# First product in plain float32 with attention between its parts, gates by tanh, mixes in pairs

## What is computed

```python
# attention: keys of the last 128 positions
scores = where(mask, scale * q @ k.T + bias, -1e9)
attn = exp(scores - max(scores)); attn = attn / (sum(attn) + 1e-9)
x = attn @ v                                # (4, 576, 512) after joining the heads
# first block, w_in 512 x 1024, w_out 1024 x 512
h = maximum(x @ w_in, 0)
gate = 1 / (1 + exp(-conv3(h)))             # 3 taps around each position
x2 = (h * gate) @ moe_w_out
# second block, w_val and w_out 512 x 512
gate2 = 1 / (1 + exp(-causal_conv5(x2)))    # 5 taps, own and four before
y = (gate2 * (x2 @ w_val)) @ moe2_w_out
```

## Time and profile before

| | |
|---|---|
| median of 3 runs | 470.3 us |
| profiled execution, its own time | 470.26 us |
| its span, first to last instruction | 468.5 us |
| mean granted TensorE clock | 0.978 |
| PE, DVE, ACT, POOL busy | 94%, 68%, 63%, 18% |
| chain that ended last | PE 81%, DVE 7%, ACT 5% |

### The profile page before, as it was taken

How to read it: one execution, slowest core, us unless ns; L and a number is a source line. 1 busy time by engine, 2 the same in 40 slices (tenths; PEclk the granted TensorE clock), 3 DMA queues, 4 the chain that set the end, 5 groups by cost and what they waited for, 6 DMA issues and landing times.

```text
span 468.5 us, 9674 instructions
## 1 busy us (share of the span) xinstructions
PE 442.6 (94%) x3376; PEld 410.3 (88%) x3376; DVE 320.3 (68%) x1128; ACT 297.1 (63%) x916; POOL 82.3 (18%) x116
## 2 busy tenths in 40 slices
PE   4888579997999999999999999999999999999997
PEld 3668558996889998999889998999889998899997
DVE  7795895976685767757776667847778475847760
ACT  3686953386667975398566976488666876377132
POOL 3310990044000220013000230014000140004000
PEclk9999857999999999999999999999999999999999
DMA  8865102001211012011210112121211100010002
GB/s 212 222 199 214 45 15 78 1 1 45 69 47 38 25 46 68 27 49 46 70 45 27 37 25 67 37 62 42 57 45 44 36 2 1 2 50 2 1 14 88
DMA packets 38928, 25.81 MB, mean 55 GB/s; under 512 B 22752, under 2 KB 35040, under 8 KB 38880
## 3 DMA queue, kind: packets, MB, share of 16 engines
q1 hardware_dynamic: 38880, 25.20, 18.7%
HBM read 20.47 MB, written 4.72 MB: 54 GB/s over the span
## 4 chain that ended last, share of the span: by engine, by line
PE 81%; DVE 7%; ACT 5%; issue 2%; DMA 1%; POOL 1%; SPq 1%; DVEq 0%; ACTq 0%
PE bank L827 20%; PE bank L828 20%; PE bank L829 20%; PE bank L808 8%; PE bank L778 8%; PE bank L788 6%; DVE probs L597 1%; DMA k_all<-k_t 1%; DVE probs L565 1%; ACT conv L468 1%; DVE gate L706 1%; DVE conv L650 1%; DVE w_lo L620 1%; ACT conv L474 1%; ACT bank L459 1%
## 5 line engine op out<-in xcount | busy, mean ns | idle before, releaser
L827 PE MATMUL bank<-g_hi,w_hi 128*128 128x288 f32 x384 | 121.2, 316 | 0.0
L827 PE MATMUL bank<-x_hi,w_hi 128*128 128x290 f32 (+1 forms) x384 | 114.3, 298 | 3.7 <-DVE x_lo L640 1.4
L828 PE MATMUL bank<-g_lo,w_hi 128*128 128x288 f32 x384 | 114.0, 297 | 0.0
L828 PE MATMUL bank<-x_lo,w_hi 128*128 128x290 f32 (+1 forms) x384 | 113.6, 296 | 0.0
L829 PE MATMUL bank<-g_hi,w_lo 128*128 128x288 f32 x384 | 113.6, 296 | 0.0
L829 PE MATMUL bank<-x_hi,w_lo 128*128 128x290 f32 (+1 forms) x384 | 113.3, 295 | 0.0
L389 POOL TENSOR_TENSOR g_lo<-conv,g_hi 128x288 fp32r<-128x288 f32 x64 | 51.9, 812 | 330.7 <-ACT g_hi L482 330.7
L650 DVE SCALAR_TENSOR_TENSOR conv<-bank,taps,conv 128x288 f32<-128x288 f32 (+1 forms) x128 | 65.5, 513 | 53.6 <-ACT conv L468 53.4
L420 ACT ACTIVATE probs<-probs,neg_max 128x192 f32<-128x192 f32 (+2 forms) x144 | 62.0, 432 | 28.9 <-DVE neg_max L565 28.4
L827 PEld LDWEIGHTS bank<-x_hi,w_hi 128*128 128x128 f32 x384 | 72.4, 188 | 4.6 <-DVE conv L658 1.8
L827 PEld LDWEIGHTS bank<-g_hi,w_hi 128*128 128x128 f32 x384 | 72.8, 190 | 0.8 <-issue 0.5
(11 more groups left out here) (49 smaller groups left out, 542.9 us busy)
## 6 DMA issues: line engine op xcount, KB each, us to landing
w_raw<-panels SPq DMA_DIRECT2D x12, 512.0 KB, 5.9
y_t<-y_sb SPq DMA_DIRECT2D x32, 144.0 KB, 1.7
q_tile<-q_t SPq DMA_DIRECT2D x32, 128.0 KB, 3.0
k_all<-k_t SPq DMA_DIRECT2D x16, 256.0 KB, 3.7
v_tile<-v_tiles SPq DMA_DIRECT2D x16, 256.0 KB, 2.7
q_tile<-q_t SPq DMA_DIRECT2D x8, 64.0 KB, 2.4
k_all<-k_t SPq DMA_DIRECT2D x4, 128.0 KB, 2.6
v_tile<-v_tiles SPq DMA_DIRECT2D x4, 128.0 KB, 3.0
```

The source lines that it names most:

```text
L827: pe.matmul(out, w_hi[:, p, col:col + P], hi(k), start=start, stop=False)
L828: pe.matmul(out, w_hi[:, p, col:col + P], lo(k), start=False, stop=False)
```

## The change

Four things are done.

*First product of chunk 0.* It multiplies the unrounded rows (`x_raw`, in the place of `x_lo`) by the unrounded weights (`w_raw`) in plain float32: 32 matmuls of 290 columns for 96 float32r ones. The first three tiles are copied to `x_raw` by ACT and not split. POOL no longer rounds panels 0 to 3 at the start, and DVE splits no weights in steps. The splits come later: ACT rounds the 98 columns of rows that both chunks read (`seam_high`, beat 10) and the four panels (`w_in_high`, 1024 columns each, beats 12 to 15), POOL keeps the rests (`seam_low`, `w_in_low`, 16 pieces). POOL rounds panels 4 to 7 in beats 0 to 3, DVE keeps their rests in halves in beats 1 to 8; panels 8 and 9 are split by POOL behind the up weights, 10 and 11 in beats 10 and 14 of chunk 1.

*Attention in the up beats.* Steps 12 to 18 of batch 0 go into beats 1 to 7 of chunk 0, step 19 into beat 12. The up product of chunk 0 uses banks 0 to 3 in turn (each waits for the gated rows four groups back); its down product makes the first parts of all four groups, then the second parts.

*Gates by tanh.* The sigmoid of z is (1 + tanh(z/2))/2: `Relu` takes a scale of 0.5 (which halves h, and so z), the gate is `Tanh`, the multiplication adds 1 in a two-operation instruction; the second gate has its scale in the activation, and the output copy takes a scale of 0.5.

*Mixes in pairs.* `probs_t` has four buffers, and PE's close does nothing at even steps and two mixes at odd ones.

```diff
+T_RING = 4
+WOVEN = 7
+PLAIN = 3
+SEAM = SEQ - READ
...
+        x_raw = nc.alloc_sbuf_tensor_at("x_raw", [P, KM, SEQ], F32, offset=base + x_raw_at)
-        probs_t = [place(f"probs_t{r}", [P, 4 * P]) for r in range(2)]
+        probs_t = [place(f"probs_t{r}", [P, 4 * P]) for r in range(T_RING)]
...
+        def up_bank(c, m):
+            return UP_BANK[m] if c > 0 else m % KM
+        def down_of(c, j):
+            n = j - DOWN0
+            if c == 0 and n < KM:
+                return n % 2, n // 2
+            return n // 2, n % 2
...
+            if c == 0 and KW - WOVEN <= j < KW:
+                return FIRST + j - KW + WOVEN
+            if c == 0 and j == DOWN0:
+                return STEPS - 1
...
-                    if c == 0 and j == VAL0 + 2:
-                        run(slot, close, range(FIRST, STEPS))
...
@@ on POOL @@
             def beat(c, j, step):
+                if c == 0 and j < P_VAL - P_OUT:
+                    round_panel(P_OUT + j)
                 if c < CHUNKS and 2 <= j < KW + 2:
                     g1_low(c, j - 2)
-                if c == 0 and j < KW and j % 2 == 1:
-                    round_panel(P_OUT + j // 2)
-                if c == 0 and j in (DOWN0, DOWN0 + 4):
-                    split_panel(P_VAL + (j - DOWN0) // 4)
-                if c == 1 and j in (0, 4):
-                    split_panel(P_OUT2 + j // 4)
-
-            for n in range(P_OUT):
-                round_panel(n)
+                if c == 0 and j == KW + 2:
+                    seam_low()
+                if c == 0 and DOWN0 <= j < DOWN0 + P_OUT:
+                    w_in_low(j - DOWN0)
+                if c == 0 and j in (DOWN0 + P_OUT, DOWN0 + P_OUT + 1):
+                    split_panel(P_VAL + j - DOWN0 - P_OUT)
+                if c == 1 and j in (KW + 2, KW + 6):
+                    split_panel(P_OUT2 + (j - KW) // 4)
...
@@ on ACT @@
+            def seam_high():
+                act.wait_ge(up_done, KW)
+                act.copy(x_hi[:, :, SEAM:PLAIN * P], x_raw[:, :, SEAM:PLAIN * P]).then_inc(seam_rounded, 1)
+            def w_in_high(n):
+                act.wait_ge(up_done, KW)
+                act.wait_ge(panel_loaded[n], 16)
+                act.copy(w_hi[:, n, :], w_raw[:, n, :]).then_inc(w_in_rounded, 1)
...
-                act.activation(bank[:, 0:READ], bank[:, 0:READ], ACT.Relu).then_inc(hidden_done, 1)
+                act.activation(bank[:, 0:READ], bank[:, 0:READ], ACT.Relu, scale=0.5).then_inc(hidden_done, 1)
...
-                               ACT.Sigmoid).then_inc(gate1_done, 1)
+                act.activation(conv[n % DEPTH][:, :], conv[n % DEPTH][:, :], ACT.Tanh).then_inc(gate1_done, 1)
...
@@ on DVE @@
-                dve.tensor_tensor(conv[n % DEPTH][:, :], banks[UP_BANK[m]][:, at:at + HALF],
-                                  conv[n % DEPTH][:, :], ALU.mult).then_inc(g1_done, 1)
+                dve.scalar_tensor_tensor(out=conv[n % DEPTH][:, :], in0=conv[n % DEPTH][:, :], scalar=1.0,
+                                         in1=banks[up_bank(c, m)][:, at:at + HALF], op0=ALU.add,
+                                         op1=ALU.mult).then_inc(g1_done, 1)
...
-                if 0 <= step - STEPS + 2 * P_VAL < 2 * P_VAL:
-                    low_of_panel(step - STEPS + 2 * P_VAL)
...
+                if c == 0 and 1 <= j < 1 + 2 * (P_VAL - P_OUT):
+                    low_of_panel(j - 1)
...
@@ on PE @@
+            def close(step):
+                if step % 2 == 1:
+                    mix(step - 1)
+                    mix(step)
...
+                    if c == 0:
+                        if m == 0:
+                            pe.wait_ge(panel_loaded[P_IN + k], 16)
+                        last = pe.matmul(banks[bank][:, 0:READ], w_raw[:, P_IN + k, m * P:m * P + P],
+                                         x_raw[:, k, at:at + READ], start=first, stop=final)
...
-            walk(slot, mix, beat)
+            walk(slot, close, beat)
```

More of the change, by code:

```diff
@@ L242, in last_of_run @@
         def last_of_run(step):
-            return step % STEPS in (FIRST - 1, STEPS - 1)
+            return step % STEPS in (FIRST - 1, STEPS - 1) and step != FIRST - 1
         def chunk_of(step):
@@ L425, in slot, with turned_rows @@
             def slot(step):
+                turned_rows(step)
+                if step + LOOK - 1 < ALL_STEPS:
+                    exps(step + LOOK - 1)
+            def turned_rows(step):
                 _, t, _ = where(step)
                 act.wait_ge(turned, step + 1)
-                reach(act, mixed, step - 1)
-                to = probs_t[step % 2]
+                reach(act, mixed, step - T_RING + 1)
+                to = probs_t[step % T_RING]
                 if 0 < t < FULL:
@@ L505, in out_rows @@
                 reach(act, y_stored[n % Y_RING], 16 * (n // Y_RING))
-                act.copy(y_sb[n % Y_RING][:, :], banks[out_bank(c, m)][:, 0:HALF]).then_inc(y_kept, 1)
+                act.activation(y_sb[n % Y_RING][:, :], banks[out_bank(c, m)][:, 0:HALF], ACT.Copy,
+                               scale=0.5).then_inc(y_kept, 1)
             def beat(c, j, step):
-                if step is not None:
+                if step is not None and j < KW:
+                    turned_rows(step)
+                elif step is not None:
                     slot(step)
@@ L516, in beat @@
                     gate_rows(c, j - 1)
+                if step is not None and j < KW:
+                    exps(step + LOOK - 1)
                 if c < CHUNKS and 2 <= j < KW + 2:
                     g1_high(c, j - 2)
+                if c == 0 and j == KW + 2:
+                    seam_high()
+                if c == 0 and DOWN0 <= j < DOWN0 + P_OUT:
+                    w_in_high(j - DOWN0)
                 if c > 0 and 0 <= j - VAL0 < KM:
                     g2_high(c - 1, j - VAL0)
-                if c < CHUNKS and DOWN0 <= j < OUT0 and j % 2 == 1:
-                    x2_high(c, (j - DOWN0) // 2)
+                if c < CHUNKS and DOWN0 <= j < OUT0 and down_of(c, j)[1] == 1:
+                    x2_high(c, down_of(c, j)[0])
                 if out_of(c, j):
@@ L631, in slot @@
                 scores(kept_early(step), 1)
-                if 0 <= step - STEPS + 2 * P_VAL < 2 * P_VAL:
-                    low_of_panel(step - STEPS + 2 * P_VAL)
             def close(step):
                 _, t, hp = where(step)
-                if hp == PAIRS - 1:
+                if hp == PAIRS - 1 and step // PAIRS >= PLAIN:
                     w = width_of(t)
@@ L674, in val_rows @@
                 dve.wait_ge(gate2_done, n + 1)
-                dve.tensor_tensor(gate2[:, m, :], banks[val_bank(c, m)][:, 0:HALF], gate2[:, m, :],
-                                  ALU.mult).then_inc(g2_done, 1)
+                dve.scalar_tensor_tensor(out=gate2[:, m, :], in0=gate2[:, m, :], scalar=1.0,
+                                         in1=banks[val_bank(c, m)][:, 0:HALF], op0=ALU.add,
+                                         op1=ALU.mult).then_inc(g2_done, 1)
             def g2_low(c, m):
@@ L796, in mix @@
                     pe.wait_ge(v_loaded[tile % V_RING], 16 * (tile // V_RING + 1))
-                    reach(pe, x_lo_done, tile)
+                    tiles_left(tile)
                 pe.wait_ge(copied, step + 1)
@@ L867, in up @@
                     pe.wait_ge(y_kept, KM * (c - 2) + OUT_BANK.index(bank) + 1)
-                product(banks[bank][:, 0:READ], lambda k: (P_IN + k, m * P),
-                        lambda k: x_hi[:, k, at:at + READ], lambda k: x_lo[:, k, at:at + READ],
-                        range(KM)).then_inc(up_done, 1)
+                for k in range(KM):
+                    first, final = k == 0, k == KM - 1
+                    if c == 0:
+                        if m == 0:
+                            pe.wait_ge(panel_loaded[P_IN + k], 16)
+                        last = pe.matmul(banks[bank][:, 0:READ], w_raw[:, P_IN + k, m * P:m * P + P],
+                                         x_raw[:, k, at:at + READ], start=first, stop=final)
+                    else:
+                        if c == 1 and m == 0:
+                            pe.wait_ge(w_in_split, (k + 1) * (PANEL // PIECE))
+                        last = product(banks[bank][:, 0:READ], lambda k: (P_IN + k, m * P),
+                                       lambda k: x_hi[:, k, at:at + READ], lambda k: x_lo[:, k, at:at + READ],
+                                       [k], first=first, final=final)
+                last.then_inc(up_done, 1)
             def val(c, m):
@@ L931, in beat @@
                 if c < CHUNKS and DOWN0 <= j < OUT0:
-                    down(c, (j - DOWN0) // 2, (j - DOWN0) % 2)
+                    down(c, *down_of(c, j))
                 if out_of(c, j):
```

62 lines of the change are left out of this document (40 added, 22 removed).

## The result

| | before | changed |
|---|---|---|
| median | 470.31 us (4 runs, 468.93 to 470.8) | 453.83 us (4 runs, 453.49 to 454.09) |
| profiled execution, own time | 470.26 us | 453.9 us |
| its span | 468.5 us | 452.0 us |
| mean granted TensorE clock | 0.978 | 1.0 |

The ratio is 0.9686 (95% interval 0.9648 to 0.9723): 3.1% faster. The forecast was 448.5 us, with a range of 443 to 457.

The account below looks back on a forecast made before the run. TensorE, busy 94% of the span, bounds it; gains come from its empty time before 121 us or its own sequence. 12.9 + 0 + 9.0 = 21.9 us off 470.26 gave 448.4, forecast 448.5 us, range 443 to 457.

Parts of the forecast that it names:

- part 5: Later batches: pairing removes 30 mix blocks at 0.30 us each, 9.0 us in full; bounds 0 and 9.6.
- Part 1: First run of 12 steps: eight steps save 3.5 us, 0.7 more before the product; up product starts at 33.5 us.
- Part 2: Up product with seven steps woven in: 27 us at 3.55 us per beat, from a two-beat loop of 7.1 us.
- The rival of contention: Woven beats: DVE stops beside POOL, 4.5 us per beat instead of 3.55; 457 us in all, chance 0.17.
- Part 3: First chunk's down product: 16.6 us with a 2.5 us wait for step 19's copies; second chunk starts at 77.1.
- Part 4: Second chunk: a new lag as large as the present 2.8 us idle time; change 0, bounds +2 and -2.8.
- The second rival: Later batches: pairing gives little, the extra returns at the turn or a PE wait opens; 454.5 us, chance 0.11.
- The hidden parts: Two-input gating, table loads, scales in activations and four small memsets: hidden; PE does not wait for the loads after 121 us.
- The slower rival: Woven beats: the loop closes in one beat, 7.1 us each, 24.9 us more; 473 us, chance 0.04.

Follow-up runs that it names:

- run 7: Changed kernel with two of four plain matmuls left out in groups 1 to 7 of the first chunk's up product: 452.09 us.
- run 6: Changed kernel with DVE's subtraction of the down weights put ahead of the taps in chunk 0's woven beats: 453.35 us.
- run 8: Changed kernel with POOL's low halves of the gated rows in chunk 0 cut to 16 of 288 columns: 454.46 us.
- run 3: Changed kernel with DVE's subtraction of rows (`x_lo`) issued one slot later, at the next step's close: 451.81 us.
- run 2: Changed kernel with the pairs undone, one mix at each step again: 457.44 us.
- run 4: Changed kernel with sigmoid gates and plain multiplication in place of the tanh gates: 471.51 us.
- run 12: Changed kernel with rows subtracted one slot later, weight subtraction ahead of the taps, and mixes of steps 18 and 19 one beat later: 447.82 us.
- run 10: Changed kernel with the three edits of run 12 plus POOL's low pieces of the first weights made by columns over all four panels: 451.82 us.
- run 9: Changed kernel with the weight subtraction ahead of the taps and the mixes of steps 18 and 19 one beat later: 451.45 us.
- run 1: Kernel before with only the mixes in pairs (four copies of the turned probabilities): 466.6 us, ratio to the kernel before 0.9961.

## Why the prediction was right, and which term was mis-sized

The changed kernel is 5.3 us above the point and inside the range. The first four parts came out within 0.1 us in sum, in part by luck, since an up product 1.1 us longer than forecast was set off by a down product 0.7 shorter and a second chunk 0.5 shorter; nearly all of the 5.3 us is part 5. By the prediction's own steps:

*Part 1, the first run.* Up product at 33.72, forecast 33.5. Right, within the spread of that start from trace to trace.

*Part 2, the woven up product.* 28.71 us for 27; 0.64 of it are the turn and the scores of step 19, which the forecast counts to the next part, so by its own terms 28.07. The turns follow each other by 3.26 to 3.97 us (first at 35.78, eighth at 61.79: 26.01 / 7 = 3.72), forecast 3.55. The mechanism, a loop from turn through ACT and DVE back to the turn two beats on, holds: taking half of the plain work out gave 3.0 us of 6.8 (run 7), taking the weight subtraction out of the loop 2.3 (run 6), and cutting POOL's part to 16 columns 1.75 (run 8). Too small was DVE's share: the subtraction stood at 0.69 us in that step and took 1.05 beside POOL. PE's own work in the stage had been put too low as well, 23.5 us for 25.57 (24.93 without step 19's). The rival of contention had the cause right and its size wrong: 0.95 us a beat for the 0.25 that run 8 gives back.

*Part 3, the down product.* 15.22 us, 15.86 with step 19's turn and scores, for 16.6. The wait for step 19's copies was 1.11, not 2.5, and the low pieces came later than needed by 0.69 where they were to fit without reserve. Second chunk at 77.65, forecast 77.1.

*Part 4, the second chunk.* Forecast no change, measured 0.46 less, with the 0.69 at its start and a 1.34 us wait of a turn at 99.14 in place of the earlier idle time.

*Part 5, the later batches.* This is the term that failed: "30 x 0.30 = 9.0 us. It comes off the end in full as PE is never idle there". Measured 3.6. Two things were wrong with it. A block is worth 0.25, not 0.30 (run 3 against run 2), which takes 1.5 to 1.8 us; its price had been put together from differences of single starts and durations, and which of them was too large is not shown. And PE did become idle, for 2.5 us of recorded time: at the second step of a tile the normalising that the turn needs stands behind the rounding of the rows and DVE's `x_lo`, before the change as after it, and the pairs took away the mix that had covered this. Run 3 takes the wait away by an order of DVE's instructions alone and gets 3.9 us back. The second rival, that pairing gives little through "a PE wait" as mixes come later, with 454.5 us, is the case that came; it had 0.11 (its "as the mixes come later" is not the reason: the normalising did not come later, the turn came earlier). That the time lies inside the range is owed to a range that had been made wide for the rivals. The mistake was to argue from PE never being idle before: a delay of half a microsecond on a side path is invisible while the mix covers it, and the change took the cover away.

*The hidden parts.* Two-operation gating and scales cost nothing in the later batches (run 2's stage); the memsets were not tried alone. The tanh gates were costed at nothing beyond being what lets exponentials and gates alternate; run 4 puts 17.7 us on that.

*The slower rival*, beats of 7.1 us, needed DVE to normalise only after the same beat's taps. DVE's order in the woven beats has the slot first, and no beat took over 4 us.

## What to carry to other kernels

An engine that is never idle before a change says nothing about the waits that its own work covers: when instructions of it are merged or moved, list for each moved one who waited for it, and what the waiting engine does next. Once the waiting is found, the cheapest cure is often the order on the engine behind, here one subtraction a slot later, for 3.9 us. And gains at several places add up only as far as each resource in between had slack: run 12's three did, run 10's fourth took 4.0 us back, as it made POOL wait for four roundings instead of one.

## What the runs showed of the hardware

*A short pause of PE can cost twice.* In the traces of runs 3, 6 and 8, with a wait of 1.75, 1.75 and 1.68 us for step 19's copies, the granted clock then stood at 0.50 for about 3.4 us, in run 6 from 1.5 us after PE had gone on, while it worked without a gap; behind one of 1.11, 0.99 or 0.17 us at that place (changed kernel, runs 7 and 9) it stayed at 1.00. The length of the pause does not decide it alone: behind one of 1.84 us in run 1 (turn at 112.37) the clock stayed at 1.00 too. Such a stretch cost 1.5 us (run 6), about as much as the pause. In the list of runs the sign of it was a mean clock of 0.996 where 1.000 was to be had.

*Some of DVE's instructions stand still beside POOL's.* An addition on two elements a partition takes 0.16 us; where POOL's low half ran from 44.62 to 45.61 it took until 45.63. DVE's and POOL's rows:

```profile
41.70 0.16 DVE L644 TENSOR_SCALAR guarded<-total 128x2 f32<-128x2 f32 x1
...
44.86 0.77 DVE L644 TENSOR_SCALAR guarded<-total 128x2 f32<-128x2 f32 x1
```

```profile
44.62 0.99 POOL L433 TENSOR_TENSOR g_lo<-conv,g_hi 128x288 fp32r<-128x288 f32 x1 [9.73 <-ACT g_hi L541]
```

With POOL's instruction shortened to 16 columns the 512-column subtraction fell from 1.05 to 0.68 us (run 8). The taps, which read a PSUM bank, took 0.51 in both. The Trainium skill, SBUF — State Buffer, section "SBUF: two separate sides", says that the loser of the shared port stands still for the other's whole instruction; these rows agree. It cost 0.25 us a beat here (1.75 us in seven, run 8) and not the 0.95 of the prediction's rival.

*Entering and leaving 64-column products.* With and without a block of mixes in stages otherwise equal but for DVE's order (runs 2 and 3), PE takes 0.25 us per block (7.2 us for 29), beside the mixes' own work.
